# Storing attention sums as 2 KB rows, and splitting half of the feed-forward input weight one stage later

## The reference, cut to what matters

```python
# attention: 4 batches, 8 heads, 768 tokens, head size 48
for t in range(S):
    cur = einsum('bhd,bhe->bhde', u * k[t], v[t])
    y[t] = einsum('bhd,bhde->bhe', r[t], state + cur)
    state = w * state + einsum('bhd,bhe->bhde', k[t], v[t])
# feed-forward, x is 3072 tokens x 384
h = x @ w_in              # 384 x 2048
g = h - tanh(h)
x = g @ w_out             # 2048 x 384
# eight experts, each token goes to its best one
out[mask] = gate_w[mask] * (relu(x[mask] @ w1[e]) @ w2[e])
```

## Time and profile before

| what | value |
|---|---|
| median of 3 runs | 868.36 us (864.88 to 868.91) |
| the profiled execution: its time | 869.71 us |
| its span, first to last instruction | 867.9 us |
| attention | 0 to about 124.4 us of the span |
| feed-forward, with routing | about 124.4 to 556 us |
| TensorE busy | 837.9 us (97%), mean granted clock 0.989 of full |
| VectorE busy | 567.5 us (65%) |
| ScalarE busy | 483.3 us (56%) |
| GpSimd busy | 286.7 us (33%) |
| DMA | 180.01 MB in 98602 packets, mean 207 GB/s |

### The profile page before, as it was taken

How to read it: one execution, slowest core, us unless ns; L and a number is a source line. 1 busy time by engine, 2 the same in 40 slices (tenths; PEclk the granted TensorE clock), 3 DMA queues, 4 the chain that set the end, 5 groups by cost and what they waited for, 6 DMA issues and landing times. The chain is left out here.

```text
span 867.9 us, 19097 instructions
## 1 busy us (share of the span) xinstructions
PE 837.9 (97%) x5568; PEld 738.4 (85%) x5569; DVE 567.5 (65%) x887; ACT 483.3 (56%) x1072; POOL 286.7 (33%) x319
## 2 busy tenths in 40 slices
PE   7999999999999999999999999999999999999995
PEld 6766768888998998998998998888999899989984
DVE  7999949999999999999999997522112111211120
ACT  4766676667778777777877866033323332333231
POOL 4555632222434433433443232212322222222211
PEclk8999999999999999999999999899999999999998
DMA  8999952116867878877877886298886476511100
GB/s 207 272 280 277 295 153 71 48 53 202 286 229 254 279 232 263 263 245 249 282 231 239 271 305 229 86 344 303 333 304 215 172 278 214 207 43 42 39 2 1
DMA packets 98602, 180.01 MB, mean 207 GB/s; under 512 B 9707, under 2 KB 24189, under 8 KB 98560
## 3 DMA queue, kind: packets, MB, share of 16 engines
q1 hardware_dynamic: 84320, 163.87, 57.9%
q0 software_dynamic: 3968, 10.82, 3.7%
q10 hardware_dynamic: 10272, 4.79, 2.6%
HBM read 114.96 MB, written 65.86 MB: 208 GB/s over the span
## 5 line engine op out<-in xcount | busy, mean ns | idle before, releaser
L1127 POOL TENSOR_TENSOR ew_l<-ew_raw,ew_h 128x512 fp32r<-128x512 f32 x96 | 126.5, 1325 | 215.0 <-DVE poly L1343 210.7
L1044 PE MATMUL y_ps<-wout_h,g_h 128*128 128x392 f32 x384 | 131.5, 343 | 3.2 <-ACT x_sb L1244 2.8
L1046 PE MATMUL y_ps<-wout_h,g_l 128*128 128x392 f32 x384 | 130.4, 340 | 0.0
L1045 PE MATMUL y_ps<-wout_l,g_h 128*128 128x392 f32 x384 | 130.3, 339 | 0.0
L1497 DVE TENSOR_TENSOR ex_hT_l<-e_bank,ex_hT_h 128x512 fp32r<-128x512 f32 x62 | 39.9, 686 | 125.3 <-ACT ex_hT_h L1653 125.3
L1044 PE MATMUL h_ps<-xT_h,win 128*128 (+1 forms) x288 | 113.3, 394 | 3.0 <-DVE diff L1324 2.1
L1046 PE MATMUL h_ps<-xT_h,win 128*128 (+1 forms) x288 | 113.3, 393 | 0.0
L1045 PE MATMUL h_ps<-xT_l,win 128*128 (+1 forms) x288 | 112.8, 392 | 0.0
L1224 ACT ACTIVATE g_h<-poly 128x512 fp32r<-128x512 f32 x96 | 61.3, 638 | 85.7 <-DVE poly L1343 85.2
L1653 ACT ACTIVATE ex_hT_h<-e_bank 128x512 fp32r<-128x512 f32 x62 | 33.8, 597 | 120.2 <-PE e_bank L1567 116.1
L1532 POOL DMA_INDIRECT out_dram<-ex_o_sb,put_i x31 | 31.1, 1002 | 203.3 <-ACT ex_o_sb L1637 203.3
(11 more groups left out here) (186 smaller groups left out, 1840.1 us busy)
## 6 DMA issues: line engine op xcount, KB each, us to landing
ew_raw<-in_w SPq DMA_DIRECT2D x96, 256.0 KB, 3.2
w_h<-ew_h SPq DMA_DIRECT2D x96, 256.0 KB, 3.5
w_l<-ew_l SPq DMA_DIRECT2D x96, 256.0 KB, 2.6
w_ex<-w_h SPq DMA_DIRECT2D x14, 1536.0 KB
w_ex<-w_l SPq DMA_DIRECT2D x14, 1536.0 KB
kv_sb<-in_kv SPq DMA_DIRECT2D x24, 384.0 KB, 12.4
krT_sb<-in_krT SPq DMA_DIRECT2D x40, 192.0 KB, 11.5
x_dram<-xt_sb ACTq DMA_DIRECT2D x48, 96.0 KB, 11.4
```

Of the source, the lines that this page charges most:

```text
L1044: pe.matmul(out, lh, rh, start=start, stop=False)
L1045: pe.matmul(out, lh, rl, start=False, stop=False)
L1046: return pe.matmul(out, ll, rh, start=False, stop=stop)
L1127: pool.tensor_tensor(ew_l[:, slot, :], raw, ew_h[:, slot, :].bitcast(F32), ALU.subtract).then_inc(ew_l_made, 1)
```

## The change

1. `x_dram` gets the shape (chunk, 2 x 48, batch, pair, 128). A store of 48 partitions now writes runs of 512 floats (2 KB). `load_group` reads them back in six DMAs, in runs of 128 floats (512 bytes), instead of one DMA with runs of 2 KB.
2. `w_in` is laid out in two halves of 1024 columns. Attention loads and splits only the first, in one piece a chunk (loaded at b = 2, high part at b = 3, low part behind `rk` of b = 1 in the next chunk). The buffer `raw` has one slot.
3. The second half comes in 8 pieces of 384 columns in group 0 of the feed-forward stage, in steps 0 to 7, each behind a piece of `w_out`. TensorE waits for the pieces from step 8 on.
4. The load of the first expert's weights follows the new layout of the columns that it overwrites; its sizes stay.

```diff
             def load_group(eng, g):
-                eng.dma_start(xg_sb, x_dram[g].rearrange("(a p) t -> p a t", p=P)).then_inc(xg_loaded, 16)
+
+                for q in range(PAIRS):
+                    at, end = q * 2 * D, (q + 1) * 2 * D
+                    while at < end:
+                        a, p = at // P, at % P
+                        n = min(end - at, P - p)
+                        src = x_dram[g, at - q * 2 * D:at - q * 2 * D + n, :, q, :]
+                        eng.dma_start(xg_sb[p:p + n, a, :].rearrange("p (b t) -> p b t", b=B), src).then_inc(xg_loaded, 16)
+                        at += n
...
-                        if b >= 2:
-                            wait(sp, low_made, 2 * c + b - 3)
-                            sp.dma_start(raw[:, b - 2, :], w_in[c, b - 2]).then_inc(raw_loaded[b - 2], 16)
-                        elif not is_first(c) and not last:
+                        if b == 2:
+                            wait(sp, low_made, c)
+                            sp.dma_start(raw[:, :], w_in[:, c * PIECE:(c + 1) * PIECE] if isinstance(c, int)
+                                         else w_in[:, bass.ds(c * PIECE, PIECE)]).then_inc(raw_loaded, 16)
+                        elif b < 2 and not is_first(c) and not last:
...
-                        if b < 2 and not is_first(c):
-                            low(c - 1, b)
+                        if b == 1 and not is_first(c):
+                            low(c - 1)
...
                     for s in range(2):
-                        act.dma_start(x_rows[c, s, :, :, b, :],
+                        act.dma_start(x_dram[c, s * D:(s + 1) * D, b, :, :],
                                       x_sb[s * HI:s * HI + D, b, :, :]).then_inc(x_stored[b], 16)
...
-                        if b >= 2:
-                            wait_apart(act, passed_act, (raw_loaded[b - 2], 16 * (c + 1)))
-                            act.activation(piece_of(c, b - 2, win_h_flat), raw[:, b - 2, :], ACT.Copy).then_inc(high_made, 1)
+                        if b == 3:
+                            wait_apart(act, passed_act, (raw_loaded, 16 * (c + 1)))
+                            act.activation(piece_of(c, win_h_flat), raw[:, :], ACT.Copy).then_inc(high_made, 1)
...
         def pieces_at(g, last, f):
 
-            if pieces(g, last) == KF:
+            if is_first(g):
+                return [2 * f, 2 * f + 1] if f < IN_LATE else [f + IN_LATE]
+            if last:
                 return [f]
...
+        def in_piece_of(f, a):
+
+            return ((a * HALF + f % HALF + 1) * P - 1) // DM * 2 + 1
+
+        def first_half(j, half):
+
+            return in_part(win[:, half, :], j) if is_in(j) else (wout_h, wout_l)[half][:, out_row(j), 0:DM]
...
                         pool.wait_ge(ew_h_made, j + 1)
-                        pool.tensor_tensor(wout_l[:, j, 0:DM], raw[:, 0:DM], wout_h[:, j, 0:DM].bitcast(F32),
+                        pool.tensor_tensor(first_half(j, 1), raw[:, 0:DM], first_half(j, 0).bitcast(F32),
                                            ALU.subtract).then_inc(ew_l_made, 1)
...
+                        if is_first(g) and f >= HALF:
+                            pe.wait_ge(ew_l_made, in_piece_of(f, a) + 1)
+                        cols = slice(f % HALF * P, (f % HALF + 1) * P)
+                        last = products(pe, h_ps[f % 2][:, :], win_h[:, f // HALF, a, cols], win_l[:, f // HALF, a, cols],
...
-                        act.activation(wout_h[:, j, 0:DM], raw[:, 0:DM], ACT.Copy).then_inc(ew_h_made, 1)
+                        act.activation(first_half(j, 0), raw[:, 0:DM], ACT.Copy).then_inc(ew_h_made, 1)
```

More of the change, by code:

```diff
@@ L47 @@
 PIECE = 512
+GROUP_LOADS = 6
+IN_LATE = 8
 NPIECE = E * 2 * KD * FE // PIECE
@@ L143, in build @@
                          wl_done, table_in, xt_sb, xt_stored, ident, consts, bank7, win, w_ex, w_out, w_logit,
-                         sumsq, w12, w12_h, w12_l, rows_sb, get_row, put_row, expert_at, ends_at, gathered,
+                         sumsq, w_in, w12, w12_h, w12_l, rows_sb, get_row, put_row, expert_at, ends_at, gathered,
                          first_loaded)
@@ L166, in attention @@
         k_sb, v_sb = (kv_sb[:, :, i, :] for i in range(2))
-        raw = sb("raw", [P, 2, PIECE])
+        raw = sb("raw", [P, PIECE])
         woT_sb = sb("woT_sb", [P, KD, FF])
@@ L221, in attention @@
         loaded = [sem(f"loaded{b}") for b in range(B)]
-        raw_loaded = [sem(f"raw_loaded{i}") for i in range(2)]
+        raw_loaded = sem("raw_loaded")
         scaled = sem("scaled")
@@ L731, in feed_forward @@
     x2_tiles = x2_dram.rearrange("(b c p) d -> b c p d", b=B, p=P)
-    win_h = win[:, 0, :].rearrange("p (a f) -> p a f", a=KD)
-    win_l = win[:, 1, :].rearrange("p (a f) -> p a f", a=KD)
+    win_h, win_l = (win[:, i, :].rearrange("p (s a f) -> p s a f", s=2, a=KD) for i in range(2))
+    HALF = KF // 2
     NP = 2 * KD * FE // PIECE
@@ L1004, in pieces, with is_in, out_row, out_piece @@
         def pieces(g, last):
-            return KF if last or (isinstance(g, int) and g == 0) else KF + EXTRA
+            return KF if last else KF + IN_LATE if is_first(g) else KF + EXTRA
         def pieces_at(g, last, f):
-            if pieces(g, last) == KF:
+            if is_first(g):
+                return [2 * f, 2 * f + 1] if f < IN_LATE else [f + IN_LATE]
+            if last:
                 return [f]
             return [f + f // EXTRA] + ([f + f // EXTRA + 1] if f % EXTRA == EXTRA - 1 else [])
+        def is_in(j):
+            return j < 2 * IN_LATE and j % 2 == 1
+        def out_row(j):
+            return j // 2 if j < 2 * IN_LATE else j - IN_LATE
+        def out_piece(f):
+            return 2 * f if f < IN_LATE else f + IN_LATE
+        def in_part(x, j):
+            at = WIDE + j // 2 * DM
+            return x[:, at:at + DM]
+        def in_piece_of(f, a):
+            return ((a * HALF + f % HALF + 1) * P - 1) // DM * 2 + 1
+        def first_half(j, half):
+            return in_part(win[:, half, :], j) if is_in(j) else (wout_h, wout_l)[half][:, out_row(j), 0:DM]
         def before(g):
-            return 0 if isinstance(g, int) and g == 0 else KF + (KF + EXTRA) * (g - 1)
+            return 0 if is_first(g) else KF + IN_LATE + (KF + EXTRA) * (g - 1)
         def uses(g, ring):
-            return 0 if isinstance(g, int) and g == 0 else KF // ring + (KF + EXTRA) // ring * (g - 1)
+            return 0 if is_first(g) else (KF + IN_LATE) // ring + (KF + EXTRA) // ring * (g - 1)
         def stores(g):
@@ L1058, in load_piece @@
                     if is_first(g):
-                        sp.dma_start(ew_raw[:, slot, 0:DM], w_out[j * P:(j + 1) * P, :]).then_inc(ew_loaded[slot], 16)
+                        src = in_part(w_in, j) if is_in(j) else w_out[out_row(j) * P:(out_row(j) + 1) * P, :]
+                        sp.dma_start(ew_raw[:, slot, 0:DM], src).then_inc(ew_loaded[slot], 16)
                     else:
@@ L1094, in load_first @@
                         sp.wait_ge(ew_l_stored[i], 16 * (NP // MADE + 1))
+                    part, at = quarter // 2, quarter % 2
                     for half, src in enumerate((w12_h, w12_l)):
-                        dst = w[:, 0, half, :].bitcast(F32).rearrange("p (a q f) -> p a q f", a=KD, f=PIECE)[:, :, quarter, :]
-                        sp.dma_start(dst, src[0:NP].rearrange("(a q) p f -> p a q f", a=KD)[:, :, quarter, :]
-                                     ).then_inc(first_loaded, 16)
+                        dst = w[:, 0, half, :].bitcast(F32).rearrange("p (s a q f) -> p s a q f", s=2, a=KD, f=PIECE)
+                        pieces_from = src[0:NP].rearrange("(s a q) p f -> s p a q f", s=2, a=KD)
+                        sp.dma_start(dst[:, part, :, at, :], pieces_from[part, :, :, at, :]).then_inc(first_loaded, 16)
                 for i in range(MADE):
@@ L1717 @@
         "u": in_columns(inputs["u"]),
-        "w_in": by_piece(inputs["moe_w_in"]),
+        "w_in": by_half(inputs["moe_w_in"]),
         "w_out": np.ascontiguousarray(inputs["moe_w_out"]),
```

46 lines of the change are left out of this document (19 added, 27 removed).

## The result

| | before | after |
|---|---|---|
| median of 10 runs | 866.6 us (863.85 to 868.91) | 870.95 us (869.19 to 876.53) |
| ratio, 95% interval | | 1.0062 (1.0038 to 1.0085) |
| the profiled execution: time, span | 869.71, 867.9 us | 876.53, 874.8 us |
| its mean granted clock | 0.989 | 0.981 |

The change costs 866.6 x 0.0062 = 5.4 us (3.3 to 7.4). The median of 10 runs before lies 1.8 us under the median of 3 that the prediction started from. The forecast was +2.8 us.

What follows compares the result with a forecast made beforehand. It took VectorE, held up by GpSimd's subtractions and `kv` waits, to bound attention, and VectorE to pace group 0. -4.4 - 0.6 + 7.8 = +2.8 us on 868.36 gave 871.2 us, range 864 to 876.

Steps and rivals of the forecast that it cites:

- Group 0, +7.8: Feed-forward group 0, steps 0 to 7: GpSimd's second subtraction holds VectorE for 0.98 us in each of 8 steps, 7.8 us.
- `g_l` would move by 0.98 us: Group 0, step 3: GpSimd is busy until 143.56, and `g_l`, ending 0.54 us behind it, comes 0.98 us later.
- TensorE has no room left: Group 0: TensorE's product follows VectorE's read of `h_ps` at 0.3 us, so each microsecond VectorE loses is lost to TensorE.
- Attention, -5.0: Attention: removing one subtraction in four tiles gives -4.4 us over four chunks, and the first chunk another -0.6 us.
- The cap of 7.4 us: Attention, 16 tiles: at most 75.26 - 16 x 4.24 = 7.4 us can be won, as TensorE's pace is 4.24 us a tile.
- 0.6 for all that lies outside the 16 tiles: Attention's first chunk, which held two such subtractions: 0.6 us won, a little under one meeting.
- The first, that the pieces cost nothing: Group 0: the load of x or the pieces cost nothing, only the -5.0 us is left, 863.4 us; chance 0.12.
- The second, in which attention wins nothing: Attention: `rk` meets `ksrs` and `kst` in every tile at 1.09 us, only 0.6 us is won, 875.6 us; chance 0.15.
- The third, that the 512-byte stores were no burden: Attention: DMAs gain only 4.6 us, half of the `kv` waits stay, 3.1 us is won, 873.1 us; chance 0.13.
- The fourth, the cap: Attention reaches its bound of -8 us, against +7.8 in group 0: 868.2 us, no change; chance 0.15.
- `g_l` near 2.0 us: Sign in the changed profile: in group 0, steps 0 to 7, VectorE's `g_l` takes near 2.0 us.
- the end of attention near 119: Sign in the changed profile: the attention stage ends near 119 us, with four tiles in 17.0 to 18.0 us.

Runs made afterwards that it cites:

- before_wait: The kernel before, with GpSimd in group 0 waiting for VectorE's last operation of the step: 862.69 us, ratio 0.9958.
- before_again: The kernel before, run once more without an edit for a second profile: 866.26 us, ratio 0.9995.
- half_only: The kernel after with the old layout, store and load of `x_dram`, so only half of `w_in` is moved: 871.1 us, ratio 1.0052.
- rows_wait: The kernel before with the new `x_dram` layout, and GpSimd in group 0 waiting for VectorE's last operation of the step: 863.12 us, ratio 0.9944.
- after_again: The kernel after, run once more without an edit: 873.44 us, ratio 1.0061.
- half_wait: The kernel after with the old `x_dram` layout, and GpSimd in group 0 waiting for VectorE's last operation of the step: 866.19 us, ratio 0.9997.
- rows_again: The kernel before with only the new `x_dram` layout, its store and six-DMA load, in a later run on another chip: 866.99 us, ratio 0.9998.

## Why the prediction was right or wrong

**Direction and size.** The forecast was +2.8 us with a range of -4.4 to +7.6 around 868.36. Measured are +5.4 (3.3 to 7.4), inside the range but over the 4.3 us that the text called the least that can be told. The median, 870.95, is near the 871.2 that was named only because the 3 runs shown lay 1.8 us above the median of 10; as a difference the forecast was 2.6 us too low.

**Group 0, +7.8 against +6.2.** The mechanism was right and the term too large: 8 x 0.98, where six steps cost 0.80 to 0.84 and the first two 0.53 and 0.78. The step that failed is "`g_l` would move by 0.98 us". `g_l` did not move. It got in between the two subtractions, and the loss fell on the next operation with two SBUF inputs, which the text had named as the other way it could go without pricing it. Here that way is cheaper. As predicted, `g_l` would have ended 0.54 us behind a second subtraction of 1.03 us, at 142.45 + 1.03 + 0.54 = 144.02, and L1376 0.60 us later (the distance at which these operations follow each other), at 144.62. It ended at 144.47, 0.15 earlier, which is the difference between 0.98 and 0.83.

**"TensorE has no room left" was a wrong reading.** The row has TensorE's product 0.3 us behind the read of `h_ps` that releases it. That says that TensorE waits for VectorE, not that it is full. Here it did no harm, as either way a microsecond of VectorE is one of TensorE. It would have hidden the 4.8 us that before_wait found. Counting the products (61 us in the 64.7 that TensorE takes from its first product of the group to the next group's) would have shown it.

**Attention, -5.0 against about -0.4.** The means of the first read of `h_ps` over all profiles are:

| | profiles | mean |
|---|---|---|
| old stores, all of `w_in` in attention | 3 | 126.0 |
| old stores, half moved | 3 | 123.2 |
| long rows, all of `w_in` | 3 | 127.4 |
| both parts | 4 | 125.6 |

The moved half alone wins 2.8 us, and the long rows give 1.4 to 2.4 back. Three steps of the working failed:

1. The cap of 7.4 us. Half of it could not be had: the first 5 of the 16 tiles in the earlier trace rows take 55.36 - 30.46 = 24.90 us, 3.7 more than at 4.24, and no kernel shortened them (24.9 to 25.8 us in the three with the moved half alone). They hold the start of the loop and a pause of TensorE's that every profile has (last section). Only the 11 tiles behind them had something to give, 50.36 - 46.64 = 3.7 us.
2. The base. These 3.7 us are of one execution, the slow one of three (first reads at 127.9, 125.2 and 124.9). In before_again the 11 tiles take 47.4 us, so the gain to be had was 0.8, and in before_wait they take 46.6 and there was none. With the change they do go at 4.24 us, and `kst` fell from 921 to 581 ns on average. But in the same view of the kernel after VectorE waits 7.3 us for TensorE's `upd`, where it had waited nothing: it got back what it could not use.
3. What was not in the sum: a tile at the low clock, 7.17 us in place of 4.24 in the given profile, so 2.9 us. It came in three of four profiles with both parts.

The 2.8 us that the moved half alone does win in the means are 1.2 before tile 4 (it starts at 29.3 in place of 30.5 us), 1.5 in the 11 tiles (46.6 in place of 48.1) and 0.5 behind them, less 0.4 in tiles 4 to 8. The prediction had 0.6 for all that lies outside the 16 tiles.

The terms then add up to -0.4 + 6.2 = +5.8 us beside the measured 5.4. The errors of the two terms, 4.6 too good and 1.6 too dear, partly cancelled, and that the forecast came as near as it did is in part luck.

**The rivals.** The first, that the pieces cost nothing, is out (74.6 us in every profile with two full subtractions and no wait). The second, in which attention wins nothing (+7.2), has that outcome right by another mechanism: not `rk` meeting `ksrs`, but no need for what was freed. The third, that the 512-byte stores were no burden, is the nearest in its number (+4.7), and its 3.1 us for the moved half alone are close to the 2.8 found. Its reason is not the one that the rows show: the stores' time on the DMA engines was saved (7.7 us on each, reckoned 6.5), and bought nothing. The fourth, the cap, falls with the cap.

**What was to be seen.** Right: steps at 5.1 us, q10 under 7000 packets, a DMA share under 1.05, hardly a wait of `kst` (0.3 us), four tiles in 17 us, groups 1 to 5 unchanged, and with them the load of x in six DMAs at no cost. Wrong: `g_l` near 2.0 us, and the end of attention near 119, that is a first read near 123. half_only alone has it there (122.91).

## What to carry to other kernels

When two engines alternate, a small distance between them says which one waits, not that the other is full: count the work of each in the stage. A gain that rests on the pace of a stage wants that pace from more than one execution, for here the 4.58 us a tile of one profile were 4.31 in the next of the same kernel. Where a helper engine's operation can block another's, its place inside the step is worth more than its length, up to the gap that it fits in: one wait on a semaphore took 4.8 us off group 0 of the kernel before and 8.3 off that of the kernel after, where leaving out nearly all of the second subtraction took 6.2.

## What the runs showed of the hardware

**Who pays between two engines that share the way to SBUF.** Two subtractions back to back did not act as one block. In the step of group 0 VectorE's `g_l`, which had been held by the first, went ahead of the second and held that one for about 0.45 us (1.47 in place of 1.03). In the earlier trace rows two pieces in group 1 ran 2.54 us without such a gap. The traces show what decides: which of the two was there first when the first subtraction ended. Two pairs of the kernel before in group 1, first the second subtraction of each, then VectorE:

```profile
213.61 1.28 POOL L1127 TENSOR_TENSOR ew_l<-ew_raw,ew_h 128x512 fp32r<-128x512 f32 x1
...
230.28 1.84 POOL L1127 TENSOR_TENSOR ew_l<-ew_raw,ew_h 128x512 fp32r<-128x512 f32 x1
```

```profile
213.65 1.79 DVE L1334 TENSOR_TENSOR g_l<-poly,g_h 128x512 fp32r<-128x512 f32 x1
...
230.28 0.68 DVE L1334 TENSOR_TENSOR g_l<-poly,g_h 128x512 fp32r<-128x512 f32 x1
230.88 1.78 DVE L1339 SCALAR_TENSOR_TENSOR poly<-quad,poly 128x512 f32<-128x512 f32 x1
```

At 213.61 `g_l` came 0.04 us too late and waited for the whole second subtraction. At 230.28 both began together, `g_l` went through, and GpSimd and the operation behind `g_l` paid. The 13 profiles hold 259 such pairs with a `g_l` at hand. In 178 its record starts 0.04 us or more behind that of the second subtraction, and it always waits. In the other 81 it starts earlier, or at most 0.01 us later, and always goes first. In these two places both ways cost the same, a step of 4.98 us.

**A low clock near 50 us, whose cause stays open.** Every profile of every kernel has a pause in TensorE's instruction stream in tile 7, at some point between 46.7 and 50.8 us, in which it waited for no engine. In the kernel after, on TensorE:

```profile
48.49 0.27 PE L691 MATMUL y<-am,kv_sb 128*48 128x128 f32 x1 [1.75 <-issue]
```

In five of seven profiles with the long rows (yes in the table, and the given one) the granted clock went to 0.50 for most of the following tile; in none of six with the old stores did it. The cost is about 3 us each time: tiles 7 and 8 together take 13.6 to 13.9 us with it and 10.5 to 10.9 without. A sixth profile with the long rows, rows_wait, has such a fall earlier, in tile 4. TensorE's stream paused there for 1.17 us, and the 13 products behind the pause took 1.62 us, where 13 such products take 0.93 in after_again:

```profile
33.24 1.62 PE L692 MATMUL y<-am,kv_sb 128*48 128x128 f32 x13 [1.17 <-issue]
```

```profile
33.52 0.93 PE L691 MATMUL y<-am,kv_sb 128*48 128x128 f32 x13 [1.46 <-issue]
```

Neither the length nor the place of the pause sorts the profiles. half_only and half_wait paused from 47.1 and 47.2 us on and kept the full clock. rows_again paused latest and shortest of all, for 1.2 us from 49.6 on, and lost it. Seven profiles against six make a link with the long rows likely, and no run was made that sets the pause alone, so how the one leads to the other was not shown.
